# An attention and two feed-forward layers on one core: the whole program rewritten, with new host layouts and another split of the elementwise work

## The reference

```python
# q, k, v: (4, 8, 576, 64); factor = 4; scale = 1/8
q_d = q.reshape(B, H, Sd, factor, D).mean(axis=3)        # also k_d, v_d: 144 groups of 4 tokens
out_up = np.repeat(softmax(scale * q_d @ k_d.T) @ v_d, factor, axis=2)
mask = np.abs(pos[:, None] - pos[None, :]) < factor      # each token sees 7 neighbours
out_local = softmax(where(mask, scale * q @ k.T, -1e9)) @ v
x = (out_up + out_local) as (2304 tokens, 512)
h = np.maximum(x @ moe_w_in, 0.0)                        # (2304, 2048)
x = h * h @ moe_w_out                                    # (2304, 512)
h = x @ moe2_w_in
out = (np.maximum(h, 0.0) + np.log1p(np.exp(-np.abs(h)))) @ moe2_w_out
```

## Time and profile before

| | us |
|---|---|
| median of three runs | 1040.85 |
| lowest, highest | 1040.21, 1041.78 |
| span of the profiled execution | 1041.6 |
| PE busy | 927.3 |
| VectorE busy | 801.0 |
| ScalarE busy | 422.8 |
| GpSimd busy | 370.2 |

### The profile page before, as it was taken

The page is one execution under the profiler, slowest core; times in us unless marked ns, Lnnn a source line. Parts: engine busy times, 40 slices in busy tenths (PEclk is TensorE's granted clock), DMA queues, the critical chain, the costliest instruction groups (busy, mean ns, idle before and its releaser), DMA issues.

```text
span 1041.6 us, 16705 instructions
## 1 busy us (share of the span) xinstructions
PE 927.3 (89%) x5848; PEld 858.1 (82%) x5848; DVE 801.0 (77%) x1096; ACT 422.8 (41%) x971; POOL 370.2 (36%) x233
## 2 busy tenths in 40 slices
PE   3543789799897999898999999999999999999998
PEld 3433689789796898787899998899999999999997
DVE  3799999887999878998775237877677776777765
ACT  1333334335334344343353675344353443533433
POOL 4676764457654657555576223000000000000000
PEclk9999899999999999999999999999999999999999
DMA  9982223421331314212100454001010010000000
GB/s 184 237 216 55 63 55 79 108 54 48 88 80 35 96 39 118 72 58 62 39 23 1 134 163 134 1 1 60 0 60 0 0 60 0 33 27 0 31 1 31
DMA packets 54840, 66.36 MB, mean 64 GB/s; under 512 B 4613, under 2 KB 42237, under 8 KB 54781
## 3 DMA queue, kind: packets, MB, share of 16 engines
q1 hardware_dynamic: 54780, 65.55, 23.4%
HBM read 56.09 MB, written 9.44 MB: 63 GB/s over the span
## 4 chain that ended last, share of the span: by engine, by line
PE 54%; issue 16%; DVE 13%; POOL 13%; SPq 3%; DMA 1%; ACT 1%; POOLq 0%; DVEq 0%; ACTq 0%
PE bank L1109 19%; PE bank L1120 18%; PE bank L581 9%; PE bank L553 7%; POOL g_lo L570 5%; POOL prod L321 4%; POOL prod L271 3%; DVE o L328 3%; DVE sc L276 1%; POOL w_lo L617 1%; SPq L609 1%; DVE vd L404 1%; DVE w_lo L617 1%; DVE prod L271 1%; DMA grp<-in_v 1%
## 5 line engine op out<-in xcount | busy, mean ns | idle before, releaser
L581 PE MATMUL bank<-g_hi,w_hi 128*128 128x288 f32 x512 | 156.0, 305 | 19.5 <-POOL g_lo L570 19.3
L553 PE MATMUL bank<-x_hi,w_hi 128*128 128x288 f32 x512 | 162.6, 318 | 7.2 <-DVE x_lo L373 4.0
L570 POOL TENSOR_TENSOR g_lo<-act,g_hi 128x288 fp32r<-128x288 f32 x128 | 121.5, 953 | 132.6 <-ACT g_hi L566 132.6
L553 PE MATMUL bank<-x_lo,w_hi 128*128 128x288 f32 x512 | 155.2, 303 | 0.0
L553 PE MATMUL bank<-x_hi,w_lo 128*128 128x288 f32 x512 | 154.9, 302 | 0.0
L581 PE MATMUL bank<-g_lo,w_hi 128*128 128x288 f32 x512 | 153.8, 300 | 0.0
L581 PE MATMUL bank<-g_hi,w_lo 128*128 128x288 f32 x512 | 153.5, 300 | 0.0
L321 POOL TENSOR_TENSOR prod<-sc,vt 128x1344 f32<-128x1344 f32 x48 | 117.4, 2446 | 98.9 <-DVE o L328 50.0
L1109 PE MATMUL bank<-x_hi,w_hi 128*128 128x384 f32 x384 | 129.8, 338 | 1.9 <-DVE g L1028 1.1
L1109 PE MATMUL bank<-x_lo,w_hi 128*128 128x384 f32 x384 | 129.8, 338 | 0.0
L1109 PE MATMUL bank<-x_hi,w_lo 128*128 128x384 f32 x384 | 129.7, 338 | 0.0
(11 more groups left out here) (81 smaller groups left out, 1851.0 us busy)
## 6 DMA issues: line engine op xcount, KB each, us to landing
w_raw<-in_moe_w_in SPq DMA_DIRECT2D x32, 256.0 KB, 4.0
w_raw<-in_moe_w_out SPq DMA_DIRECT2D x32, 256.0 KB, 5.0
kt<-in_k SPq DMA_DIRECT2D x30, 240.0 KB
vt<-in_v SPq DMA_DIRECT2D x30, 240.0 KB
grp<-in_q SPq DMA_DIRECT2D x32, 144.0 KB
grp<-in_k SPq DMA_DIRECT2D x32, 144.0 KB
grp<-in_v SPq DMA_DIRECT2D x32, 144.0 KB
qt<-in_q SPq DMA_DIRECT2D x32, 144.0 KB, 5.3
```

Of the source, the lines that this page charges most:

```text
L553: last = nc.tensor.matmul(h_ps[f % 2][:, 0:NT], w[:, f, wc], x[:, kc], start=(kc == 0 and i == 0), stop=(kc == KC - 1 and i == 2))
L570: nc.gpsimd.tensor_tensor(g_lo[:, f % 2], act[:, f % 2], g_hi[:, f % 2].bitcast(F32), ALU.subtract).then_inc(g_ready, 1)
L581: last = nc.tensor.matmul(y_ps[d][:, 0:NT], w[:, f, wc], g[:, f % 2], start=(f == 0 and i == 0), stop=(f == FC - 1 and i == 2))
```

## The change

The program is written anew; what is computed and the tiles stay.

- The host lays out the inputs: local q, k, v by tile over all 128 partitions (k and v with their halo), v with its tokens innermost (vt is `[P, 2, D, CW]`); group q and k with d over partitions and tokens innermost; group v with the four members innermost; weights of one f as one row of 1024.
- Group sums (pool_qk, pool_v) are three VectorE reduces over four neighbouring elements, q and k already transposed, so that the transposes and their copies fall away. Both heads of a pair go in one go: scores in two banks, two maxima, one scaling (dnb), exponentials out of PSUM with that bias, one norm over 72x576 elements. ScalarE copies the transposed probabilities, VectorE scales up.
- All products after the start are on GpSimd; at the start four of twelve are on VectorE. The value product keeps the window of seven innermost, and value_sum sums over these.
- hidden_lo moves from GpSimd to VectorE, first in each step.
- w_lo of the first layer: ten on GpSimd, six on VectorE within tile 0. All of the second layer's on VectorE, with W2_LAG = 2; split_x2(0) comes behind tile 7's steps.
- Loops are unrolled; one transfer of 512 KB for each weight block, one each for the local q, k, v.

```diff
-        def hidden_lo(pool, T, f):
-            pool.wait_ge(gh_ready, CREDIT_RELU + FC * T + f + 1)
-            nc.gpsimd.tensor_tensor(g_lo[:, f % 2], act[:, f % 2], g_hi[:, f % 2].bitcast(F32),
+        def hidden_lo(dve, T, f):
+            n = FC * T + f
+            dve.wait_ge(gh_ready, n + 1)
+            nc.vector.tensor_tensor(g_lo[:, f % 2], act[:, f % 2], g_hi[:, f % 2].bitcast(F32),
...
-            pb = sc[:, e, TC * c:TC * c + TC, :].unsqueeze(3).to_broadcast([P, TC, WIN, D])
-            nc.gpsimd.tensor_tensor(prod[:, i % 2], pb, window(vt, e, TC * c), ALU.mult).then_inc(pv_prod, 1)
+            pb = sc[:, h, TC * c:TC * c + TC, :].unsqueeze(2).to_broadcast([P, TC, D, WIN])
+            a = vt[:, h, 0:1, TC * c:TC * c + 1]
+            win = bass.AP(a.tensor, a.offset, [a.ap[0], [1, TC], [CW, D], [1, WIN]])
+            dst = prod[:, m % 2].rearrange("p (t d w) -> p t d w", t=TC, d=D)
+            e.tensor_tensor(dst, pb, win, ALU.mult).then_inc(prod_ready[m % 2], 1)
...
-            nc.vector.tensor_reduce((qd, kd, vd)[x][:].rearrange("g m h d -> g (m h) d"),
-                                    grp[:, x].rearrange("g m h f d -> g (m h) d f"),
-                                    AX_X, ALU.add).then_inc(grp_sum, 1)
+            nc.vector.tensor_reduce(qp[:], qs.rearrange("p (g f) -> p g f", f=FACTOR), AX_X,
+                                    ALU.add).then_inc(qk_pooled, 1)
+            nc.vector.tensor_reduce(kp[:], ks.rearrange("p (g f) -> p g f", f=FACTOR), AX_X,
+                                    ALU.add).then_inc(qk_pooled, 1)
...
+                for s in range(FC):
+                    if local and s == 14:
+                        local_add(dve, T + 1, 2)
+                        x_split_lo(dve, T + 1)
+                    hidden_lo(dve, T, s)
...
+                        if 3 + 3 * (T == 0) <= s < 3 + 3 * (T == 0) + NPROD:
+                            value_sum(dve, T + 1, s - 3 - 3 * (T == 0))
...
+                    if down:
+                        if s == 1:
+                            pool_v(dve, n)
+                        if s == 2:
+                            pair_max(dve, n)
+                        if s == 4:
+                            pair_norm(dve, n)
...
+                    if down and f in (3, 8):
+                        pair_exp(a, n + (f == 8))
...
+                    if f in (3, 8):
+                        pair_turn(pe, n + (f == 8))
```

More of the change, by code:

```diff
@@ L26, with build @@
 EPS = 1e-9
[L29 to L53, removed]
+B, H, S, D = 4, 8, 576, 64
+DM, FF = 512, 2048
+FACTOR = 4
+WIN = 2 * FACTOR - 1
+HALO = FACTOR - 1
+SCALE = 1.0 / float(D) ** 0.5
+NT = S // 2
+TILES = 2 * B
+NC = 32
+CT = NT // NC
+CW = CT + 2 * HALO
+TC = 3
+NTC = CT // TC
+NPROD = 2 * NTC
+KC = DM // P
+FC = FF // P
+G = S // FACTOR
+GH = G // 2
+NT2 = 384
+TILES2 = B * S // NT2
+SUB2 = NT2 // P
+def build(nc, q_loc, k_loc, v_loc, q_grp, k_grp, v_grp, w1, w2, out):
     with ExitStack() as ctx:
@@ L273, in score_sums @@
[L273 to L289 removed]
+        LO_POOL = 10
@@ L364, in x_split_hi @@
             a.wait_ge(o_T_used, NTC * (T + 1))
-            if not (isinstance(T, int) and T == 0):
+            if T > 0:
                 a.wait_ge(h_ready, FC * T)
@@ L454, in down_exp, with pair_exp, pair_norm @@
+        def pair_exp(a, n):
+            a.wait_ge(ds_max, n + 1)
+            if n:
+                a.wait_ge(dp_T, n)
+            for e in range(2):
+                for m in range(2):
+                    last = nc.scalar.activation(pd[:, e, m], pair_banks(n)[e][0:GH, m * G:m * G + G], ACT.Exp,
+                                                bias=dnb[:, e, m:m + 1], scale=SCALE / (FACTOR * FACTOR),
+                                                accum_out=dsm[:, e, m:m + 1])
             last.then_inc(ds_exp, 1)
-        def down_norm(dve, b, j, e):
-            n = 2 * (KC * b + j) + e
+        def pair_norm(dve, n):
@@ new lines, in pair_turn, with pair_turn_copy, pair_values @@
+            last.then_inc(dp_T, 1)
+        def pair_turn_copy(a, n):
+            a.wait_ge(dp_T, n + 1)
+            if n:
+                a.wait_ge(up_ps, n)
+            for e in range(2):
+                nc.scalar.activation(pdT[:, e].rearrange("g m k -> g (m k)"), pair_banks(n)[e][0:GH, 0:2 * G],
+                                     ACT.Copy).then_inc(dp_T_used, 1)
+        def pair_values(pe, n):
+            pe.wait_ge(dp_T_used, 2 * n + 2)
+            pe.wait_ge(v_pooled, n + 1)
+            for kh in range(2):
+                for e in range(2):
+                    last = nc.tensor.matmul(pair_banks(n)[0][D * e:D * e + D, 2 * G:3 * G], vd[:, kh, e],
+                                            pdT[:, e, kh], start=(kh == 0), stop=(kh == 1))
+            last.then_inc(up_ps, 1)
@@ L587, in output_copy @@
         def output_copy(a, T):
-            more = not (isinstance(T, int) and T == TILES - 1)
-            a.wait_ge(o_T, NTC * (T + (2 if more else 1)))
+            a.wait_ge(o_T, NTC * min(T + 2, TILES))
             for d in range(KC):
@@ new lines, in _ @@
+            for i in range(NPROD):
+                if NPROD + i not in FIRST_DVE:
+                    value_mult(pool, 0, i)
+            for f in range(LO_POOL):
+                weight_lo(pool, f, 0, w_lo_pool)
+                if f >= 2 and f - 2 < NPROD:
+                    score_mult(pool, 1, f - 2)
+            for T in range(TILES - 1):
+                for i in range(NPROD):
+                    value_mult(pool, T + 1, i)
+                if T + 2 < TILES:
+                    for i in range(NPROD):
+                        score_mult(pool, T + 2, i)
@@ L1008, in split_x2 @@
+            for T in range(TILES):
+                slot(T)
             def split_x2(i):
```

1075 lines of the change are left out of this document (477 added, 598 removed).

## The result

The changed kernel takes 1048.11 us (median of four runs, 1046.61 to 1048.74) against 1041.32 us for the kernel before beside it: a ratio of 1.0054, 95% interval 1.0039 to 1.0069. It is slower by half a percent. The prediction said 1034.5 us and faster; the time lies inside its range, on the wrong side of no change.

A forecast was written before the change was run, and what follows sets the result against it. VectorE operations held by GpSimd's products make PE wait: tiles stay near 70 us. 80.1 + 84.0 + 71.6 + 280.4 + 53.5 + 465.7 = 1035.3 against 1041.6; the median 0.8 lower, 1034.5 us; 8 in 10 from 990 to 1062.

The forecast's parts named there:

- start: Stretch ahead of the first tile's first matmul on g: 80.1 us against 109.7, 29.6 us less.
- first tile: Tile 0: 84.0 us against 76.2, with w_lo, two more score sums and two more low clocks on top of 70.1.
- the rest: Tile 7 with the second layer: 457.7 us plus net 8 for the second layer's entry, 465.7 us.
- the walked tile: A middle tile followed operation by operation: PE floor 56.4 us plus 7.7, 1.7, 2.6 and 1.7 of waits and clock, 70.1 us.
- first stall: PE waits for the first head pair's transposes of pd behind hidden_out(3): 7.7 us, plus 1.7 us of low clock.
- second stall: PE waits for the second head pair's norm, done at 43.4 us and wanted at 40.8: 2.6 us.
- the wait for x_lo: Step 14 of a tile: the last score product holds x_lo(0), wanted at 61.9 and there at 63.6: 1.7 us.
- the entry's stall: Ahead of layer two's first matmul: 6.7 us, plus 1.7 of clock and some 2.5 behind it; net 8.
- The value product: GpSimd's product with windows of seven innermost: taken at 3.05 us, bounds 2.45 and 4.0, before 2.446.
- The first rival: Slower: GpSimd's windows of seven are dear; gain gone at 3.3 us a value product, 1057 us at 4.0; chance 0.20.
- The second rival: Faster: VectorE gets in between GpSimd's products, some 4 us of wait stay, tiles of 60, 965 us; chance 0.15.
- 34% for slower: Whole kernel: 0.11 within the forecast's 12 us, 0.20 for dear windows of seven, 0.03 for value sums staying at 2.54 us.

The follow-up runs named there:

- busy PE: Changed kernel plus matmuls whose result nobody reads (80 behind hidden_out(3), 24 behind hidden_out(8), tiles 0 to 5): 1041.08 us, ratio 1.0024; runs in two groups, profile of one at 1049.1.
- statistics in PSUM: Changed kernel with the maxima (dmx) and sums (dsm) of the group softmax in PSUM instead of SBUF, order kept: 982.96 us, ratio 0.944.
- Paced: Changed kernel with only waits added on GpSimd: each product waits for VectorE's remainder of g of a given step; no work moves: 1002.38 us, ratio 0.9625.
- remainder back: Changed kernel with the remainder of g on GpSimd again, value products behind remainders of steps 1, 2, 4, 5, 7, 8; all products stay on GpSimd: 1018.2 us.
- norm first: Changed kernel with the first head pair's norm moved ahead of the value sum at step 4 of a tile: 1017.7 us, ratio 0.977.
- old division: Changed kernel with VectorE multiplying every second score product and GpSimd taking the remainder of g again, value products spread over steps 1 to 8: 1011.6 us, ratio 0.9698.
- halves of the old division: For the score products: changed kernel with VectorE multiplying every second one, the remainder of g staying on VectorE: 1042.94 us, ratio 1.0016.

## Why the prediction was wrong

**Sign and size.** The sum was 1035.3 against a span of 1046.1: 10.8 us short. By its terms: start +1.9 (82.0 for 80.1), first tile +1.3 (85.3 for 84.0), second +1.9 (73.5 for 71.6), tiles 2 to 5 +6.2 (286.6 for 280.4), tile 6 -1.5 (52.0), the rest +1.0 (466.7 for 465.7). The forecast gain of 6.3 us was smaller than these misses. The median lies 2.0 us above this span, where the prediction took it 0.8 below, so that the medians differ by 13.6.

**The step that failed** is the clock in the walked tile. The prediction gave the first stall 1.7 us for one stretch of 3.3 us at 1.2 GHz and the second stall none, and so made all tiles 70.1 us. The even ones are (70.0 and 70.1). The odd ones are 73.2 and 73.3. The clock after the second stall, which is 3.3 us long in both, in tile 2 (first two rows) and tile 3:

```profile
283.20:286.60 3.40, 3.40 (x30) 3.40 (x31) 1.70 (x2) 1.56 (x4) 1.56 (x1) 1.00 0.00 0
286.60:290.00 3.40, 3.40 (x30) 3.04 (x29) 2.43 (x3) 0.90 (x3) 1.50 (x1) 1.00 0.00 0
...
353.90:357.30 3.40, 3.40 (x18) 3.40 (x19) 1.77 (x2) 0.70 (x2) 1.49 (x1) 0.50 0.00 0
357.30:360.70 3.40, 3.40 (x18) 3.23 (x18) 0.00 (x0) 0.86 (x3) 1.57 (x1) 0.58 0.03 5
```

30 matmuls in 3.4 us at 2.4 GHz, 18 at 1.2. A stretch is 6.8 or 10.2 us in these tiles, not 3.4 as in the earlier trace rows. What it costs can be read against "busy PE", where the clock stays at 1.00. There PE takes 17.83 us from the end of the first stall to the start of the second (271.25 to 289.08) and 27.7 from the end of the second to the end of the tile. In the changed kernel tile 2 takes 19.98 and 27.7 us, tile 3 20.76 and 30.1. So the clock costs 2.2 or 2.9 us behind the first stall, where the prediction had 1.7, and none or 2.4 behind the second, where it had none. In tiles 2 to 5 that is 15.0 us for the forecast 6.8: 8.2 too few, more than the gain of 6.3 us. The misses of the start and tile 0 were not taken apart.

The price came from one wait of 3.79 us and was used for a stall of 7.7. The kernel before had shown besides that a shorter wait can have it too: PE waits 2.55 us for g_lo at 363.27, and behind it stands (columns as in the earlier trace rows)

```profile
363.30:366.60 3.30, 3.30 (x15) 3.24 (x16) 3.30 (x3) 0.49 (x2) 1.55 (x1) 0.50 0.00 0
```

That the even tiles hit 70.1 us to 0.1 is luck: the first stall and the wait for x_lo were each 0.5 us shorter than forecast, the second stall 0.7 longer and the clock 0.5 dearer.

**What was right.** The mechanism and the place: the norm behind GpSimd's products. The walk said 7.7 us for the first stall (measured 7.2), 2.6 for the second (3.3), 1.7 for x_lo (1.1 to 1.2), and L405 as the wait that ends last; value sums came out at 1.54 us, the entry's stall at 6.7 and the wait behind it at 2.4, the start 27.7 us shorter instead of 29.6. The Trainium skill, "SBUF — State Buffer", section "Who interferes with whom", says that a VectorE operation with at most one SBUF input, outside the modes that use both ports, doesn't contend with GpSimd; the runs agree (749 ns with dsm in PSUM, 1944 in SBUF).

**The value product** was taken at 3.05 us and is 3.14: 0.09 us times the four products ahead of the first stall, 0.4 us a tile at most. The first rival, which ended slower by dear windows of seven, had the sign and not the cause; its point of decision, 3.3 us, wasn't reached in the middle value. The second rival (holds miss PE) didn't happen, but "statistics in PSUM" shows what it would have been worth: 65 us.

**What was weighed badly.** The walk showed that 13 us of every tile hang on where products start, and the 34% for slower came mostly from another place. The prediction had seen that both engines fit under PE's 56.4 us by totals and not by order; it didn't name the reason, that the new GpSimd queue, with nothing between its products, had lost its only pacing. "Paced", "remainder back" and "norm first" each give back 30 to 46 us.

**Still open:** why equal stalls come with 3.4, 6.8 or 10.2 us at 1.2 GHz, or with none; what the remainder of g on VectorE costs besides the rhythm; and what of tile 0's 85 us is holds. It falls to 77.2 with the old division, and VectorE's w_lo reaches 4.2 us there against 1.2 alone, but no run took that apart.

## What to carry to other kernels

Where one engine's long instructions hold another's short ones, the rhythm counted more than the load: less work on GpSimd ("halves of the old division", the score products) brought 5 us, more work in between (the remainder) 30. So before work is moved, write down what will stand between two long instructions of the other engine, and which short operations of the chain need that gap. Small statistics that stand in a latency chain belong in PSUM when a neighbour reads SBUF all the time. Freed busy time is worth nothing until PE's longest wait is traced through it: 48 us less of VectorE's sums, bought with 33 us more of GpSimd's products, made a kernel 3 us slower.
